# Batch 0 of a decayed linear attention: decay scans over three chunks instead of one, scores as two 48-row products, range tests on ScalarE, and norm tiles 3 to 5 at other half steps

## The reference, cut to what matters

```
state = alpha[t] * state + k[t] (x) v[t];   y[t] = q[t] . state        # attention, per batch and head
x = y as [token, 384];  u = x + real(fft over tokens and channels of x)
x2 = u + relu(norm(u) @ w_ch1) @ w_ch2                                 # 384 -> 1536 -> 384
u2 = x2 + token MLP(x2);   out = u2 + relu(u2 @ w2_ch1) @ w2_ch2
```

## Time and profile before

| | |
|---|---|
| median of 3 runs | 916.11 us (915.68 to 916.67) |
| the profiled execution | 916.13 us, its span 914.3 us |
| PE busy | 888.1 us (97%) |
| DVE, ACT, POOL busy | 464.5, 311.5, 206.4 us |
| batch 0's visits | about 8 to 64 us |
| tail of batch 0 | 64 to 90.5 us |
| half steps of batches 0 to 3 | 90.5 to about 480 us |

### The profile page before, as it was taken

One profiled execution on the slowest core, in us unless ns is written; L12 is line 12 of the kernel. 1 busy time (PEld: TensorE's weight loads), 2 busy tenths in 40 slices (PEclk: granted clock), 3 DMA queues, 4 the chain that ended last, 5 costly groups with the idle time before them and its releaser, 6 DMA issues.

```text
span 914.3 us, 14646 instructions
## 1 busy us (share of the span) xinstructions
PE 888.1 (97%) x5376; PEld 855.8 (94%) x5376; DVE 464.5 (51%) x1127; ACT 311.5 (34%) x826; POOL 206.4 (23%) x360
## 2 busy tenths in 40 slices
PE   8888899999999999999999999999999999999998
PEld 5767799999999998999999999999999999999998
DVE  6887877647767558776462225222323232223121
ACT  4773455423555324554233333221121122112111
POOL 4763453202333013333013322000200020002000
PEclk9999899999999999999999999999999999999999
DMA  9904022021230040220028002000200020000000
GB/s 245 358 1 117 1 59 59 27 69 50 64 81 1 28 117 27 59 59 27 1 70 259 27 27 78 1 27 1 78 0 26 0 77 0 26 19 7 0 26 26
DMA packets 14360, 50.81 MB, mean 56 GB/s; under 512 B 1408, under 2 KB 5632, under 8 KB 12368
## 3 DMA queue, kind: packets, MB, share of 16 engines
q1 hardware_dynamic: 13728, 46.95, 16.8%
q0 software_dynamic: 576, 3.15, 0.9%
HBM read 40.66 MB, written 9.44 MB: 55 GB/s over the span
## 4 chain that ended last, share of the span: by engine, by line
PE 85%; DVE 8%; issue 2%; ACT 2%; POOL 1%; DMA 1%; DVEq 0%; SPq 0%; ACTq 0%
PE bank L1160 24%; PE bank L1162 24%; PE bank L1161 24%; PE bank L1174 4%; PE bank L1193 3%; PE bank L1198 2%; PE bank L1183 1%; DVE ext L740 1%; PE bank L1292 1%; PE bank L1404 1%; DVE suf L770 1%; DMA qkap<-qka 1%; PE bank L1168 1%; DVE stats L948 1%; DVE at L845 1%
## 5 line engine op out<-in xcount | busy, mean ns | idle before, releaser
L1035 DVE SCALAR_TENSOR_TENSOR hl<-bank,hh 128x384 fp32r<-128x384 f32 x192 | 107.0, 557 | 329.9 <-ACT hh L655 329.9
L655 ACT ACTIVATE hh<-bank 128x384 fp32r<-128x384 f32 x192 | 94.4, 492 | 349.9 <-PE bank L1162 349.6
L1160 PE MATMUL bank<-nh,w1h 128*128 128x384 f32 x288 | 102.5, 356 | 0.4 <-DVE nl L991 0.4
L1160 PE MATMUL bank<-w2h,hh 128*128 128x384 f32 x288 | 101.0, 351 | 0.2 <-DVE u L1050 0.2
L1160 PE MATMUL bank<-u2h,w3h 128*128 128x384 f32 x288 | 97.0, 337 | 0.9 <-DVE u2l L1116 0.9
L1162 PE MATMUL bank<-nh,w1l 128*128 128x384 f32 x288 | 97.4, 338 | 0.0
L1161 PE MATMUL bank<-nl,w1h 128*128 128x384 f32 x288 | 97.1, 337 | 0.0
L1160 PE MATMUL bank<-w4h,hh 128*128 128x384 f32 x288 | 96.9, 337 | 0.0
L1162 PE MATMUL bank<-w2h,hl 128*128 128x384 f32 x288 | 96.9, 337 | 0.0
L1161 PE MATMUL bank<-w2l,hh 128*128 128x384 f32 x288 | 96.6, 335 | 0.0
L1162 PE MATMUL bank<-u2h,w3l 128*128 128x384 f32 x288 | 96.3, 334 | 0.0
(11 more groups left out here) (147 smaller groups left out, 1867.6 us busy)
## 6 DMA issues: line engine op xcount, KB each, us to landing
qkap<-qka SPq DMA_DIRECT2D x15, 1008.0 KB, 6.7
vt<-v SPq DMA_DIRECT2D x16, 288.0 KB, 7.9
raw_a<-w_ch SPq DMA_DIRECT2D x6, 768.0 KB, 9.7
mid<-u SPq DMA_DIRECT2D x8, 576.0 KB, 2.8
raw_b<-w_ch SPq DMA_DIRECT2D x6, 768.0 KB, 6.0
out<-u SPq DMA_DIRECT2D x8, 576.0 KB, 2.8
xr<-mid SPq DMA_DIRECT2D x7, 576.0 KB, 3.9
raw_t<-w_tok SPq DMA_DIRECT2D x2, 768.0 KB, 5.9
```

The source lines that it names most:

```text
L655: act.activation(hh[:, s % 4, :], bank[s % 2][:, 0:HALF], ACT.Relu).then_inc(s_hhi, 1)
L1035: dve.scalar_tensor_tensor(out=hl[:, s % 4, :], in0=bank[s % 2][:, 0:HALF], scalar=0.0, in1=hh[:, s % 4, :].bitcast(F32), op0=ALU.max, op1 ...
L1160: pe.matmul(out_ap, wh, rh, start=first, stop=False)
```

## The change

In batch 0 alone, unless said otherwise:

- The layout of an input unit becomes queries, keys, then alpha with one extra zero ahead of each chunk (`HW` = 129 values per chunk), so that one scan can run over several chunks and restart at each. The restart values lie in two PSUM banks (`unit_at`, `inv_at`).
- Chunks are prepared in `PIECES`: chunk 0, chunks 1 and 2, then threes. Suffix scan, strided reciprocal and prefix scan on DVE, key and query products on POOL each cover a piece. Piece k, k+1, k+2 (k a multiple of 3) has its suffix scan and key product at visit k-5, its prefix scan and query product at visit k-4. On POOL `decay` now comes ahead of the products.
- `qz` is not used: the scores are two 48-row products, one per head, into two PSUM banks (`pairs`).
- `extreme` is replaced by `out_of_range` on ACT: a Relu with a bias and an accumulated output over the 768 values. The range test on DVE moves from visit 16 to 19, the flag from visit 18 to 23.
- The `fill` product within the visits goes; the four after the last visit stay.
- `weight_hi` at visits 9 to 19 (six) instead of 9 to 23 (eight), three before the tail, three at half step 41. `weight_lo` at visits 12, 15 and 18 (three) instead of six visits, three after the Fourier input is split, two more after `fourier_v(0)` and before the prep of batch 1, four in batch 1's visits as before.
- For all batches: `LATE_NORM_AT` from 3, 7, 14 to 6, 12, 20, and `PAUSES` to match.

```diff
-PAUSES = (0, 1, 7, 14, 22)
+PAUSES = (0, 1, 6, 12, 20)
-LOW_AT = (10, 12, 14, 16, 18, 20)
+HI_AT = (9, 11, 13, 15, 17, 19)
+HI_FOLD = 9
+LOW_AT = (12, 15, 18)
+LOW_F1 = 6
-RANGE_AT = {1: (1, 0), 2: (1, 1), 4: (0, 0), 5: (0, 1), 7: (2, 0), 8: (2, 1), 11: (3, 0), 13: (3, 1)}
+RANGE_AT = {0: (1, 0), 1: (1, 1), 4: (2, 0), 5: (2, 1), 10: (3, 0), 12: (3, 1), 14: (0, 0), 16: (0, 1)}
-LATE_NORM_AT = {3: 3, 7: 4, 14: 5}
+LATE_NORM_AT = {6: 3, 12: 4, 20: 5}
...
+            def first_visit(k):                                    # POOL
+                decay(0, k + 2)
+                if k == -2:
+                    prep_k(0, 1, 2)
+                    prep_q(0, 1, 2)
+                elif k == -1:
+                    prep_k(0, 3, 3)
+                elif k == 0:
+                    prep_q(0, 3, 3)
+                elif k % 3 == 1 and k + 5 < STEPS:
+                    prep_k(0, k + 5, 3)
+                elif k % 3 == 2 and k + 4 < STEPS:
+                    prep_q(0, k + 4, 3)
...
+                if a == 0:                                         # POOL, after fourier_v(0)
+                    pool.wait_ge(s_un[0], 2)
+                    for i in range(LOW_F1, 2 * NA - len(LATE_LOW_AT)):
+                        weight_lo(i)
...
+            def out_of_range(n, i):                                # ACT
+                if n == 0:
+                    src = alpha0[0:PR, 0:NC * HW]
+                    act.wait_ge(s_alpha2, 16)
+                else:
+                    src = qkap[n][0:PR, 2 * S:2 * S + NC * HW]
+                    act.wait_ge(*unit_loaded(0, n))
+                if (n, i) != (1, 0):
+                    act.wait_ge(s_ext, RANGED[n] - 2 + i)
+                act.activation(tested[...], decays(src), ACT.Relu, scale=(1.0, -1.0)[i],
+                               bias=limits[0:PR, i:i + 1], accum_out=ext[0:PR, i, n:n + 1]).then_inc(s_ext, 1)
...
+            def piece_suffix(i):                                   # DVE
+                k, end = PIECES[i]
+                slot, n = suf_at(k)[0], end - k
+                first = k % 3 * HW + 1
+                if i == 0:
+                    dve.wait_ge(s_alpha, 16)
+                elif k % NC == 0:
+                    dve.wait_ge(*unit_loaded(0, k // NC))
...
+                dve.tensor_tensor_scan(suf[0:PR, slot, first:first + n * HW - 1][:, ::-1],
+                                       qkap[k // NC][0:PR, at_:at_ + n * HW - 1][:, ::-1],
+                                       unit_at[0:PR, first:first + n * HW - 1][:, ::-1], 1.0, ALU.mult, ALU.add)
...
+            def piece_prefix(i):                                   # DVE
...
+                dve.reciprocal(inv_at[0:PR, first - 1:first + (n - 1) * HW:HW],
+                               suf[0:PR, slot, first:first + (n - 1) * HW + 1:HW]).then_inc(s_inv, 1)
+                if k and k % NC == 0:
+                    dve.wait_ge(s_ext, RANGED[k // NC])
...
+                dve.tensor_tensor_scan(both, both, inv_at[0:PR, first - 1:first - 1 + n * HW], 0.0, ALU.mult, ALU.add)
...
+                if a == 0:                                         # TensorE, attn_scores
+                    pe.wait_ge(s_qk, 2 * prepared(a, k))
+                    for h in range(2):
+                        mm = pe.matmul(pairs[k % 2][:, h, 0:P], k_of(a, k, head_rows(h)), q_of(a, k, head_rows(h)),
+                                       start=True, stop=True)
+                    return mm
...
             for k in range(-2, STEPS):                             # TensorE
                 visit(0, k)
-                fill(0 if k < 0 else 4 if k == STEPS - 1 else 1)
+            fill(4)
```

More of the change, by code:

```diff
@@ L62, in state_index, with piece_of @@
     return (k // NC) * (NC - 1) + k % NC
+def piece_of(k):
+    return next(i for i, (first, end) in enumerate(PIECES) if first <= k < end)
 def program(nc, qka, v, v_sizes, w_ch1, w_ch2, w_tok1, w_tok2, w2_ch1, w2_ch2, dft, cs, mask_in, ident_in, flip_in, col_in, out):
@@ L86, in program @@
     XB = NC * DM * 4
-    QB = 3 * S * 4
+    QB = QW * 4
     o_q = o
-    qkap = [sb(f"qkap{i}", [P, 3, S], o + i * QB) for i in range(2)]
+    qkap = [sb(f"qkap{i}", [P, QW], o + i * QB) for i in range(2)]
     xf = sb("xf", [P, 2 * KT, DM], o)
@@ L114, in program @@
     w4l = sb("w4l", [P, NF, DM], o_a + 3 * MB, F32R)
[L116 removed]
+    qkap += [sb(f"qkap{i + 2}", [P, QW], o + i * QB) for i in range(2)]
     nh = sb("nh", [P, KT, S], o, F32R)
@@ L514, in _ @@
             pool.wait_ge(s_xlo, 2 * KT)
-            for i in range(len(LOW_AT), 2 * NA - len(LATE_LOW_AT)):
+            for i in range(len(LOW_AT), LOW_F1):
                 weight_lo(i)
@@ L659, in _ @@
             act.activation(spare[:, 0:1], ones[:, 0:1], ACT.Sqrt).then_inc(s_spare, 1)
-            act.wait_ge(s_zero, 7)
-            wi = 0
+            act.wait_ge(s_zero, 10)
             for k in range(-2, STEPS):
                 visit(0, k)
[L664 to L667, removed]
+                if k in RANGE_AT:
+                    out_of_range(*RANGE_AT[k])
+                if k in HI_AT:
+                    weight_hi(HI_AT.index(k))
+            for i in range(len(HI_AT), HI_FOLD):
                 weight_hi(i)
@@ L671, in _ @@
                 tail(0, h)
+                if h == V_AT_LAST:
+                    for i in range(HI_FOLD, 2 * NA):
+                        weight_hi(i)
             for b in range(B):
@@ L753, in attn_state @@
                     dve.scalar_tensor_tensor(out=st[0:PR, k % 3, :], in0=st[0:PR, (k - 1) % 3, :],
-                                             scalar=suf[0:PR, k % RING, 0:1], in1=kv_of(a, k), op0=ALU.mult, op1=ALU.add
+                                             scalar=chunk_decay(k), in1=kv_of(a, k), op0=ALU.mult, op1=ALU.add
                                              ).then_inc(s_st, 1)
-            def nothing(a):
-                return zero_col if a == 0 else zeros[0:PR, 0:1]
             def prep_suffix(a, k):
[L763 to L771, removed]
+                slot, first = suf_at(k)
@@ L775, in prep_inverse @@
-                dve.wait_ge(s_suf, a * STEPS + k + 1)
-                dve.reciprocal(inv[0:PR, j:j + 1], suf[0:PR, j, 0:1]).then_inc(s_inv, 1)
+                dve.wait_ge(s_suf, prepared(a, k))
+                dve.reciprocal(inv[0:PR, k % RING:k % RING + 1], chunk_decay(k)).then_inc(s_inv, 1)
             def prep_prefix(a, k):
[L779 to L782, removed]
-                    dve.wait_ge(s_ext, a * (2 * NU) + (2 * (k // NC + 1) if a else RANGED[k // NC]))
@@ L1197, in attn_back @@
                         pe.wait_ge(s_dec[h], a * STATES + state_index(k - 1) + 1)
-                    mm = pe.matmul(y, buf[0:PR, 0, cols], dec[0:PR, k % 3, :], start=False, stop=True)
+                    mm = pe.matmul(y, q_of(a, k), dec[0:PR, k % 3, :], start=False, stop=True)
                 return mm
```

232 lines of the change are left out of this document (157 added, 75 removed).

## The result

The kernel after takes 928.2 us (median, 927.8 to 929.8 in four executions), the kernel before beside it 916.3 (915.7 to 916.7): a ratio of 1.013 (95% interval 1.012 to 1.015; the ratios below are also to the kernel before, executed beside each run). Slower, where I forecast 903.8 and said 0.92 for faster. The profiled execution took 927.87, its span 926.1.

What follows compares the result with a forecast made beforehand. DVE was taken to bound batch 0's visits, TensorE almost everything from 103 us; 916.1 - 13.5 (visits) + 0.3 + 0.4 (first seam) + 0.5 (seams two and three) = 903.8 us; 50% for 902 to 906, eight in ten 899.5 to 909.5.

Steps and rivals of the forecast that it cites:

- The `fill` goes (0.45): Batch 0's visits: without the `fill` product TensorE needs 0.45 us less in each visit.
- a rival with its price, 929: Batch 0's visits: without `fill` the clock may fall after ACT's wait at visit 2; all 19 visits +25, 929 us; 5%.
- TensorE, nearly full afterwards, would get the clock back: Batch 0's visits, argument against a fallen clock: new idle time only 1.8 us, then a nearly full TensorE restores the clock.
- my 1.6 (28.8 for 18): Batch 0's visits 4 to 21: 12 with an ACT pass at 1.65 us and 6 at 1.5, 28.8 us.
- my 50.5: End of batch 0's visits, where the tail's first `fill` begins: 50.5 us in place of 63.99, 13.5 gained.
- DVE, ACT, POOL: Batch 0's visits: three-chunk scans 0.95 and 1.02 us, POOL's products 0.9 to 1.25, ACT's range test 0.75 to 0.95.
- not 15.2: Visit 0 of batch 0: ACT waits for unit 1, whose `vt` lands at 15.2 us.
- Two 48-row products at no cost: Batch 0's visits: two 48-row score products take TensorE no longer than before; bounds 0.2 us less, 0.4 more.
- my rival had 0.35: Batch 0's visits: products of unlike row counts can't overlap, 0.35 us in each of 21 visits, 911.2 us; 12%.
- Tail, cost 0: Tail behind batch 0's visits: TensorE sets the time and it moves unchanged, cost 0; up to 0.7 us if the flag is late.
- First seam, +0.3 and +0.4: Before batch 1's scores: +0.3 us for the norm tile at half step 6, +0.4 for DVE's scan delayed beside POOL's `weight_lo`.
- the other two seams: Seams two and three: the moved norm tile only lengthens idle time, +0.25 us each, +0.5.

Runs made afterwards that it cites:

- e18: Kernel after, no fill, with the buffers from `us` on moved up by 192 bytes: 925.3 us, ratio 1.010.
- e5: Kernel after with fill products at visits 0 to 3 alone (1, 3, 2, 1): 906.0 us with the clock held, 916.1 where it fell; ratio 0.994.
- e6: Kernel after with one fill product behind visits 0 to 21, but three at visit 1 and two at visit 2: 912.0 us, ratio 0.996.
- e7: Kernel after with one fill product behind visits 0 to 21 and both score products over 112 rows instead of 48: 909.7 us, ratio 0.995.
- e15: Kernel after with e6's fills, buffers up by 960 bytes, and POOL's two `weight_lo` again ahead of batch 1's preparation: 911.9 us, ratio 0.995.
- e4: Kernel before with only norm tiles 3, 4 and 5 moved to half steps 6, 12 and 20, pauses to match: 916.1 and 916.9 us, ratio 1.000.
- e13: Kernel after with e6's fills and the buffers from `us` on moved up by 192 bytes: 908.6 us, ratio 0.992.
- e11: Kernel after with e6's fills and the buffers from `us` on moved up by 64 bytes: 912.5 us, ratio 0.997.
- e8: Kernel before with all buffers behind `nl` moved 64 bytes further on: 919.6 us, ratio 1.004.
- e9: Kernel after, no fill, with both score products over 112 rows instead of 48: eight executions from 904.5 to 926.9 us.
- the 911.5: One execution of the kernel after with one fill product behind visits 0 to 21: 911.5 us; others of that kernel took 912.1, 947.2 and 947.6.

## Why the prediction was wrong

- *The fill's removal, "The `fill` goes (0.45)".* The step that failed. I counted it as TensorE time saved; it was what kept the clock: without it TensorE ran at 1.2 GHz for 58 us, and visits 4 to 21 took 47.5 us instead of 28.8. I had the mechanism as a rival with its price, 929 (measured 928.2), its place (after ACT's wait; PE idled 1.32 and 0.61 by 15.3) and the visit at 1.2 GHz (2.9 for a full one; measured 2.82), and gave it 5%. That 929 is so near is partly luck: some 3 us of the 928.2 are the place of `hh` and `hl`, which the rival did not have (e18: 925.3). What made it 5% was the sentence that TensorE, nearly full afterwards, would get the clock back. It was full from 20 us on and stayed at 1.2 GHz until 73.7. "TensorE: Matmul & The Clock Gate" of the Trainium skill, Part 1, has a busy TensorE return to 2.4 GHz; by that the clock would have come back early in the visits. The trace differs (5.00 of 5 us busy at clock 0.50, ten stretches long): busy time in the profile is not what decides. The one piece of evidence that I had, that the kernel before held its clock in these visits with a fill in each, I did not weigh.
- *The visits.* At full clock they are as forecast: in e5, without fill, twelve visits take 18.45 us (scores at 20.72 to scores at 39.17), 1.54 each, against my 1.6 (28.8 for 18). In the kernel after visits 4 to 21 take 47.5 us (19.70 to 67.22), 2.64 each: 18.7 of the 20.5 us by which the tail's first `fill` (70.98) misses my 50.5. The rest is 0.8 until visit 4 and 1.0 behind visit 21.
- *DVE, ACT, POOL.* Scans over three chunks 0.96 (forecast 0.95 and 1.02), POOL's products 0.91 to 0.96 (0.9 to 1.25), the range test 0.94 with a separate 0.19 behind it, which overlap: 0.93 from its start to the next instruction's (14.06 to 14.99; 0.75 to 0.95). Unit 1 landed at 14.06, not 15.2.
- *Two 48-row products at no cost.* Wrong by 0.16 a visit (e6 against e7), some 3 us in all at full clock; my rival had 0.35.
- *Tail, cost 0.* 1.3 us, since its first fills still ran at 1.2 GHz.
- *First seam, +0.3 and +0.4.* 0.3 together: the scan beside `weight_lo` took 0.69 instead of 0.42, and e15 gives 0.23 of it back. For the other two seams I had +0.5; the lag changed by -0.3 and 0. That is no sign that the tile is free: 0.36 of it is the stretch at 1.2 GHz, which ended earlier after the first scores, and e4 shows the tile's 0.3.
- *Not in the sum:* the place of `hh` and `hl`. With 192 bytes e18 is 2.9 us faster than the kernel after, e13 3.4 to 3.8 faster than e6 and e11, and e8 3.9 slower than the kernel before. The prediction has no term for it. Together the misses are 20.5 + 1.3 - 0.4 - 0.7 + 3.4 = 24.1 us, the distance from 903.8 to the profiled 927.9.

No run reached 903.8. The nearest with nothing left out are 905.7 (half the fills and the place restored) and e5's 906.0, which held its clock with the place not restored. Less e18's 2.9 the latter would be 903, an estimate that no run tried.

## What to carry to other kernels

A dummy product that looks like waste may hold TensorE's clock: before taking it out, look at what else in that stretch would, and do not count on a busy engine to win the clock back. Look at the granted clock by stretch before the groups, and repeat a run: with its clock at 0.996 or at 0.955 one kernel gave 911 and 947. When a buffer ahead of others grows, note where the streamed operands land; here 64 bytes cost 0.4% of the time, far from the edit.

## What the runs showed of the hardware that I had not expected

- TensorE counted as busy for 5.00 of 5 us stretch after stretch and stayed at 1.2 GHz for 58 us; in e9's trace, with 112-row products, it came back after some 27. What in the work decides this, the runs do not say beyond fill and rows.
- An execution with fills and a low clock is dearer than one without fills (947 against 928). No trace of it was kept; an estimate from the two means of the clock gives some 78 us at 1.2 GHz beyond those of the 911.5, against 57 for the kernel after.
- Passing between 48 and 112 or 128 rows costs 0.08 to 0.09 us. Products in different row groups were not seen side by side: two of them (four instructions) took 0.43, as much as over 112 rows.
- In the last channel MLP a product of 128x384 whose streamed operand lies at remainder 0 or 192 of 256 bytes took 338 ns, at 128 it took 334; in the earlier one it took 336 at 128 and at 192.
- ACT's accumulated output is read by an instruction of its own, 0.19 us long; the next pass started 0.93 us after the start of the one that lasted 0.94, so most of it was hidden.
